# Strassen's seven-product scheme for the two MLP products over pairs of batches, with attention in head pairs and transposed activations

## The chip, the cores and the metric

The kernel runs on one NeuronCore of one Trainium2 chip. The metric is the device time of one execution in microseconds (us); lower is better. TensorE (PE in the profile) multiplies matrices: it loads a stationary tile of weights and streams a moving tile of up to 448 columns here into PSUM. VectorE (DVE), ScalarE (ACT) and GpSimd (POOL) work element by element; DVE and ACT read PSUM. SyncE (SP) only starts transfers in this kernel.

## The reference

Attention over 4 batches, 12 heads, 448 positions and 64 channels per head, then two MLP blocks on the 448x768 activations of each batch. Only the first MLP has a layer norm; the second has a low-rank mixing over the sequence in front of it.

```python
def _attn_ref(q, k, v, g_q, g_k):
    q_n, k_n = (rmsnorm(q, g_q), rmsnorm(k, g_k))
    scores = scale * np.matmul(q_n, k_n.transpose(0, 1, 3, 2))
    attn = softmax(scores)
    return np.matmul(attn, v)
def _moe_ref(x, g_ln, w_ch1, w_ch2):       # w_ch1 768x3072, w_ch2 3072x768
    xn = (x - mu) / np.sqrt(var + 1e-06) * g_ln
    return x + np.maximum(xn @ w_ch1, 0.0) @ w_ch2
def _moe2_ref(x, U, V, w_ch1, w_ch2):      # U 448x32, V 32x448
    u = x + (x.transpose(0, 2, 1) @ U @ V).transpose(0, 2, 1)
    return u + np.maximum(u @ w_ch1, 0.0) @ w_ch2
```

## The kernel before

Precision: each factor of a large product is split into a high part in the format fp32r and the low remainder (`x_hi`, `x_lo`), and a product is the sum of three matmuls, hi x hi, hi x lo and lo x hi. ACT makes a high part by a copy, DVE the low part by a subtraction.

**Attention** (function `attention`) goes head by head, 48 heads, in a loop over pairs of heads whose body `step` is written out for each engine with fixed offsets between the stages (a software pipeline). For each head PE does: 4 transposes of the normalised k (`turn_k`, L333), 4 times two matmuls for the scores (`score`, L296 and L297; q's high and low half are stacked into 128 rows, so two matmuls replace three), 16 transposes of the exponentials (`turn_exp`, L308) and 16 fp32 matmuls with v (`values`, L322; the trace has two records for each). DVE takes the row maxima (`maximum`, L444), the bias (`scale_max`, L452), k's low part (L469), q's low part (L476), half of the copies of the transposed exponentials (`copy_et`, L463), the sums of squares (L486) and the scaled output (L505). ACT does the exponentials (L372), the other copies and the high parts. POOL squares q and k (`square`, L249), takes the power -0.5 (L267) and normalises k (L271). The result stays in SBUF (`x_all`), natural layout: positions on the partitions.

**MLPs** (function `mlps`) run in 8 stages, one batch of one MLP each. A stage needs its input with channels on the partitions: `build_item` (L669) transposes it, ACT and DVE split it into `in_hi` and `in_lo` (L786, L851, L854). The 3072 hidden channels are 24 blocks of 128. For block j, `hidden` (L733) does 6 x 3 matmuls of 128x128 by 128x448 into one PSUM bank, ACT and DVE make `h_hi` and `h_lo` of it (L817, L932), and `output` (L750) does another 6 x 3 that add to six PSUM banks kept for the whole stage. PE computes block j+1's `hidden` ahead of block j's `output`. Weights come from memory for each block (`load_weights`, L98 and L99), and are split by ACT (L781, L782) and DVE (L844, L845) in tiles of 128x768, three blocks ahead. At a stage's end the six banks are copied (`y_out`, L812 and L927), transposed back in the next stage (`back_item`, L680), and added to x (`residual`, L891). The low-rank mixing stands in the stages 1 to 4 (L698, L706). POOL has three instructions in this part. Each engine runs its own list in the order in which it is written; semaphores hold an instruction until what it reads is there.

## Time and profile before

| | |
|---|---|
| device time, median of 3 runs | 1796.21 us (1795.0 to 1798.2) |
| span of the profiled execution | 1794.6 us |
| first matmul of the first MLP stage | at 344.56 us |
| last matmul of the last `output` | at 1784.44 us |
| busy share of PE, DVE, ACT, POOL | 98%, 51%, 39%, 11% |
| matmul records | 10272 |

The span is read as attention up to 344.56 us, the eight stages from there to 1784.44 us (1440 us), and 10 us for the last transposes, sums and stores. Busy shares are an average over these parts. In attention DVE is busy nearly all the time as well; in the MLPs it is so for some 40%.

### The profile page before, as it was taken

To read this page: it belongs to the slowest core of one execution; us is meant where nothing else is said; L and a number is where in the kernel's file an instruction comes from. 1 tells how busy PE (TensorE), PEld (TensorE's weight loads), DVE (VectorE), ACT (ScalarE), POOL (GpSimd) and SP (SyncE) were. 2 spreads that over 40 slices of the span, in tenths; PEclk is the share of its full clock that TensorE was granted. 3 is DMA by queue.
4 is the path that set the end of the run, shared out by engine and by line. 5 is a ranking of instruction groups with operands and counts; after the bars stand their busy time and mean duration, and the time that the engine had idled before them with its cause. 6 is when DMAs were issued, how large, how long until landed. Compare 5 with 4: busy or idle time off the path is not lost.

```text
span 1794.6 us, 29017 instructions
## 1 busy us (share of the span) xinstructions
PE 1766.4 (98%) x10272; PEld 1655.9 (92%) x10272; DVE 913.4 (51%) x1595; ACT 706.3 (39%) x1268; POOL 202.1 (11%) x201
## 2 busy tenths in 40 slices
PE   6999999999999999999999999999999999999998
PEld 5999999899999999999999999999999999999997
DVE  7999999743344444444444444444433433343332
ACT  5777777522333323332333233323222322232221
POOL 6666666000000000000000000000000000000000
PEclk9999999999999999999999999999999999999999
DMA  2222224233333233333333333332433333333320
GB/s 73 69 69 72 68 71 139 87 106 116 113 106 103 93 111 101 106 106 106 105 108 100 102 100 106 106 106 89 138 121 106 97 131 121 106 99 128 121 88 31
DMA packets 205744, 180.41 MB, mean 101 GB/s; under 512 B 12497, under 2 KB 179281, under 8 KB 205649
## 3 DMA queue, kind: packets, MB, share of 16 engines
q1 hardware_dynamic: 203280, 173.51, 30.3%
q10 hardware_dynamic: 2368, 5.51, 0.8%
q8 instruction: 75, 1.23, 0.3%
q14 instruction: 21, 0.16, 0.0%
HBM read 173.48 MB, written 5.51 MB: 100 GB/s over the span
## 4 chain that ended last, share of the span: by engine, by line
PE 80%; DVE 0%; issue 0%; ACT 0%
PE h_ps L733 39%; PE y_ps L750 38%; PE h_ps L680 1%; PE h_ps L669 1%; PE h_ps L698 1%; PE h_ps L706 0%; PE y_ps L658 0%; DVE in_nat L891 0%; ACT in_hi L786 0%; DVE in_lo L854 0%; DVE in_lo L851 0%; DVE y_t L927 0%
## 5 line engine op out<-in xcount | busy, mean ns | idle before, releaser
L844 DVE TENSOR_TENSOR w_lo<-w_raw,w_hi 128x768 fp32r<-128x768 f32 x190 | 182.0, 958 | 674.0 <-ACT w_hi L782 674.0
L750 PE MATMUL y_ps<-h_hi,w_hi 128*128 128x448 f32 x1152 | 424.4, 368 | 0.0
L733 PE MATMUL h_ps<-in_hi,w_hi 128*128 128x448 f32 x1152 | 415.9, 361 | 3.1 <-DVE in_lo L851 1.1
L733 PE MATMUL h_ps<-in_hi,w_lo 128*128 128x448 f32 x1152 | 417.9, 363 | 0.0
L750 PE MATMUL y_ps<-h_hi,w_lo 128*128 128x448 f32 x1152 | 417.8, 363 | 0.0
L750 PE MATMUL y_ps<-h_lo,w_hi 128*128 128x448 f32 x1152 | 417.7, 363 | 0.0
L733 PE MATMUL h_ps<-in_lo,w_hi 128*128 128x448 f32 x1152 | 417.4, 362 | 0.0
L781 ACT ACTIVATE w_hi<-w_raw 128x768 fp32r<-128x768 f32 x189 | 159.7, 845 | 538.1 <-PE y_ps L750 538.1
L817 ACT ACTIVATE h_hi<-h_ps 128x448 fp32r<-128x448 f32 x192 | 104.7, 545 | 380.1 <-PE h_ps L733 338.5
L733 PEld LDWEIGHTS h_ps<-in_hi,w_hi 128*128 128x128 f32 x1152 | 215.6, 187 | 19.1 <-DVE in_lo L851 1.5
L733 PEld LDWEIGHTS h_ps<-in_lo,w_hi 128*128 128x128 f32 x1152 | 216.2, 188 | 15.8
L750 PEld LDWEIGHTS y_ps<-h_lo,w_hi 128*128 128x128 f32 x1152 | 216.7, 188 | 14.0
L750 PEld LDWEIGHTS y_ps<-h_hi,w_hi 128*128 128x128 f32 x1152 | 215.9, 187 | 13.5
L750 PEld LDWEIGHTS y_ps<-h_hi,w_lo 128*128 128x128 f32 x1152 | 216.1, 188 | 13.0
L733 PEld LDWEIGHTS h_ps<-in_hi,w_lo 128*128 128x128 f32 x1152 | 216.1, 188 | 12.4
L845 DVE TENSOR_TENSOR w_lo<-w_raw,w_hi 128x768 fp32r<-128x768 f32 x190 | 180.7, 951 | 0.0
L322 PEld LDWEIGHTS av_ps<-v_nat,e_t 112*112 112x112 f32 x1536 | 172.7, 178 | 5.2
L322 PE MATMUL av_ps<-v_nat,e_t 112*112 112x64 f32 x1536 | 174.2, 257 | 0.0
L782 ACT ACTIVATE w_hi<-w_raw 128x768 fp32r<-128x768 f32 x189 | 156.4, 827 | 0.0
L932 DVE SCALAR_TENSOR_TENSOR h_lo<-h_ps,h_hi 128x448 fp32r<-128x448 f32 x192 | 118.9, 619 | 71.6 <-ACT h_hi L817 70.9
L372 ACT ACTIVATE e_nat<-scores,nbias,rs_all 112x448 f32<-112x448 f32 x192 | 138.0, 721 | 40.3 <-DVE nbias L452 40.2
L444 DVE TENSOR_REDUCE nmax<-scores 112x1 f32<-112x448 f32 x192 | 113.2, 615 | 4.3 <-PE scores L297 1.6
(90 smaller groups left out, 1407.3 us busy)
## 6 DMA issues: line engine op xcount, KB each, us to landing
w_raw<-in_moe_w_ch SPq DMA_DIRECT2D x384, 384.0 KB, 3.8
qk_raw<-in_q SPq DMA_DIRECT2D x48, 112.0 KB, 2.0
qk_raw<-in_k SPq DMA_DIRECT2D x48, 112.0 KB, 2.1
qt_raw<-in_q_t SPq DMA_DIRECT2D x48, 112.0 KB, 2.5
v_nat<-in_v SPq DMA_DIRECT2D x48, 112.0 KB, 2.0
out<-o_nat ACTq DMA_DIRECT2D x12, 336.0 KB, 5.0
out<-in_nat ACTq DMA_DIRECT2D x4, 336.0 KB, 3.1
...
```

Of the source, the lines that this page charges most:

```text
L322: last = nc.tensor.matmul(av_ps[:TP, m * D:(m + 1) * D], e_t[:, m, c, :], v_nat[:, slot, c, :], start=(c == 0), stop=(c == NI - 1))
L372: nc.scalar.activation(e_nat[:, i, :], scores[i][:TP, :S], ACT.Exp, bias=nbias[:, i:i + 1], scale=rs_all[:, ds(g, 1), i:i + 1].rearrange(" ...
L444: nc.vector.reduce_max(nmax[:, i:i + 1], scores[i][:TP, :S], axis=AX, negate=True).then_inc(rawmax_done, 1)
L669: last = nc.tensor.transpose(h_ps[c % 2][:, i * TP:(i + 1) * TP], in_nat[:, i, c * P:(c + 1) * P], ident[:TP, :TP])
L733: last = nc.tensor.matmul(h_ps[j % 2][:, :S], w[:, j % NW, c, :], x[:, c, :], start=(c == 0 and t == 0), stop=(c == DC - 1 and t == 2))
L750: last = nc.tensor.matmul(y_ps[c][:, :S], w[:, j % NW, c * P:(c + 1) * P], x[:, j % 2, :], start=(j == 0 and t == 0), stop=(j == FC - 1 an ...
L781: nc.scalar.activation(w1_hi[:, r], w1_raw[:, r], ACT.Copy)
L782: nc.scalar.activation(w2_hi[:, r], w2_raw[:, r], ACT.Copy).then_inc(w_hi_done, 1)
L817: nc.scalar.activation(h_hi[:, j % 2, :], h_ps[j % 2][:, :S], ACT.Relu).then_inc(hhi_done, 1)
L844: nc.vector.tensor_tensor(w1_lo[:, r], w1_raw[:, r], w1_hi[:, r].bitcast(F32), ALU.subtract)
L845: nc.vector.tensor_tensor(w2_lo[:, r], w2_raw[:, r], w2_hi[:, r].bitcast(F32), ALU.subtract).then_inc(w_lo_done, 1)
L932: nc.vector.scalar_tensor_tensor(h_lo[:, j % 2, :], h_ps[j % 2][:, :S], 0.0, h_hi[:, j % 2, :].bitcast(F32), ALU.max, ALU.subtract).then_i ...
```

## The change

The kernel is rewritten as one function without hardware loops.

**Attention in head pairs.** A step n of 96 takes one quarter of the positions for both heads of a pair. q and k of the two heads lie on the partitions 0 to 63 and 64 to 127. The scores are three terms (hi x hi, hi x lo, lo x hi) of two matmuls each, one on the rows of each head (`score`, L682). One DVE instruction takes the maxima of both heads (L980). The squares, the power and k's normalisation are done once for a pair on POOL, with twice the elements, and POOL now makes q's low part too (L555). DVE adds the layer-norm statistics and the normalisation (L1016, L1034) in this part; PE transposes x and, if needed, the normalised x into the channel layout (`turn_x`, L713), and the results go to scratch tensors in memory (`xres`, `xnrm`). The first stage's inputs are made in the steps 67 to 94. Only six steps overlap with the MLPs.

**MLPs in 4 stages of two batches.** The two batches are the two column blocks of the right matrix, two halves of the contraction its row blocks, and two halves of the output channels the row blocks of the left one: 2x2 blocks, which Strassen's scheme multiplies with 7 block products instead of 8. `G` products (hidden layer) have 3 chunks x 3 terms = 9 matmuls, `M` products (second layer) 2 x 3 = 6. A stage has 12 groups of 7 `G` products and 18 of 7 `M` products; in a cycle of the order 14 `G` products and 21 `M` products alternate, and each stage has six such cycles. Two `G` products of the next pair of groups (`HEAD`) stand ahead of the `M` products. Matmuls of this kind: 6048, against 6912 before.

The scheme needs sums of blocks. Sums of weights (4 for each group, `weight_sum`, L601), of the input (`make_sums`, L568 to L578) and of the hidden layer (`hidden_sums`, L608 to L618) are done on POOL. Then high and low parts of seven weight, seven input and seven hidden blocks are made, ACT the high and DVE the low ones. Products are combined after each from PSUM by DVE: `combine` (five for each `G` group) and `gather` (seven for each `M` group, into `acc` and `u_acc` in SBUF). Six PSUM banks rotate; P2, P3 and P4 are added by PE onto the banks of P1, P5 and P7 once these have been read out. x and the output keep the channel layout, so the transposes of the MLP stages go; the mixing transposes its tiles in the stages 1 and 2 (L748 to L764). Weights are loaded once for two batches.

```diff
@@ the order of the products @@
+P1, P7, P6, P5, P2, P3, P4 = range(7)
+ORDER = {"G": (P1, P7, P6, P5, P2, P3, P4), "M": (P1, P5, P6, P2, P7, P3, P4)}
+ONTO = {P2: P1, P3: P5, P4: P7}
+        for j in range(NJ):
+            for g in (2 * j, 2 * j + 1):
+                prods += [("G", s, g, k) for k in ORDER["G"][HEAD if g == 2 * j and j else 0:]]
+            if j + 1 < NJ:
+                prods += [("G", s, 2 * j + 2, k) for k in ORDER["G"][:HEAD]]
+            prods += [("M", s, j * NM + m, k) for m in range(NM) for k in ORDER["M"]]
@@ PE @@
-                    nc.tensor.matmul(scores[i][:TP, :S], lhs, k_hi[:, slot, :], start=True, stop=False)
-                    nc.tensor.matmul(scores[i][:TP, :S], lhs, k_lo[:, slot, :], start=False,
-                                     stop=True).then_inc(scores_done, 1)
+                    for a, b in ((q_hi, k_hi), (q_hi, k_lo), (q_lo, k_hi)):
+                        for h in range(2):
+                            rows = slice(h * D, (h + 1) * D)
+                            last = nc.tensor.matmul(mm_ps[:TP, 2 * (n % 2) + h, :S], a[rows, t % 2, i * TP:(i + 1) * TP],
+                                                    b[rows, t % 2], start=a is q_hi and b is k_hi, stop=a is q_lo)
+                def product(q):
+                    kind, s, n, k = prods[q]
+                    pe.wait_ge(wlo_done, q + 1)
+                    if before[q] is not None:
+                        read_out(pe, before[q])
...
+                    if kind == "M" and n % NM == 0:
+                        pe.wait_ge(hlo_done, cut(s * NG + 2 * (n // NM) + 1, k))
...
+                        for p, (w, x) in enumerate(((w_hi, x_hi), (w_hi, x_lo), (w_lo, x_hi))):
+                            last = nc.tensor.matmul(bank(q), w[:, q % RING, c * P:(c + 1) * P], x[:, k, c],
+                                                    start=k not in ONTO and c == 0 and p == 0,
+                                                    stop=c == chunks - 1 and p == 2, skip_group_check=k in ONTO)
@@ POOL @@
+                def weight_sum(r, k):
...
+                    if k == P5:
+                        out, in0, in1, op = s1, a21, a22, ALU.add
...
+                    if k == P6:
+                        out, in0, in1, op = s2, s1, a11, ALU.subtract
...
+                    nc.gpsimd.tensor_tensor(out, in0, in1, op).then_inc(sum_done, 1)
+                def hidden_sums(q):
...
+                        nc.gpsimd.tensor_tensor(t_t1, t_c12, t_b11, ALU.subtract).then_inc(th_done, 1)
+                        pool.wait_ge(th_done, 4 * g + 1)
+                        nc.gpsimd.tensor_tensor(t_c12, t_c22, t_t1, ALU.subtract).then_inc(th_done, 1)
@@ DVE @@
-                nc.vector.tensor_tensor(w1_lo[:, r], w1_raw[:, r], w1_hi[:, r].bitcast(F32), ALU.subtract)
-                nc.vector.tensor_tensor(w2_lo[:, r], w2_raw[:, r], w2_hi[:, r].bitcast(F32),
-                                        ALU.subtract).then_inc(w_lo_done, 1)
+                def weight_low(q):
+                    dve.wait_ge(whi_done, q + 1)
+                    w = width(q)
+                    nc.vector.tensor_tensor(w_lo[:, q % RING, :w], weights(q), w_hi[:, q % RING, :w].bitcast(F32),
+                                            ALU.subtract).then_inc(wlo_done, 1)
+                def hidden_low(g, k):
+                    dve.wait_ge(hhi_done, cut(g, k))
...
+                    nc.vector.tensor_tensor(h_lo[:, k, g % 2], src, h_hi[:, k, g % 2].bitcast(F32), ALU.subtract
+                                            ).then_inc(hlo_done, 1)
+                def combine(q):
...
+                        nc.vector.tensor_tensor(t_c22, bank(q), t_c22, ALU.add).then_inc(comb_done, 1)
+                def gather(q):
...
+                    dve.wait_ge(prod_done, q + 1)
...
+                    nc.vector.tensor_tensor(to, bank(q), to, ALU.add).then_inc(ev_done, 1)
```

On PE, in attention, part of one head stood like this before (scores of one head between the values and transposes of its neighbours; `scores`, `et_ps`, `av_ps` are PSUM tiles):

```order
L322 MATMUL av_ps<-v_nat,e_t 112x64 x4
L296 MATMUL scores<-k_hi,q_st 112x448
L297 MATMUL scores<-k_lo,q_st 112x448
L308 MATMUL et_ps<-ident,e_nat 112x112 x4
L322 MATMUL av_ps<-v_nat,e_t 112x64 x4
L333 MATMUL kt_ps<-ident,kn 128x112 x4
L296 MATMUL scores<-k_hi,q_st 112x448
L297 MATMUL scores<-k_lo,q_st 112x448
L322 MATMUL av_ps<-v_nat,e_t 112x64 x4
L308 MATMUL et_ps<-ident,e_nat 112x112 x8
```

On PE, in the middle of attention, one step stands like this now, up to the next step's scores (`mm_ps` holds scores and values, `sc_ps` the transposes):

```order
L682 MATMUL mm_ps<-k_hi,q_hi 112x448 x2
L682 MATMUL mm_ps<-k_lo,q_hi 112x448 x2
L682 MATMUL mm_ps<-k_hi,q_lo 112x448 x2
L702 MATMUL mm_ps<-v,e_t 112x64 x4
L690 MATMUL sc_ps<-ident,e_nat 112x112 x4
L702 MATMUL mm_ps<-v,e_t 112x64 x4
L690 MATMUL sc_ps<-ident,e_nat 112x112 x4
L713 MATMUL sc_ps<-ident,x_nat 128x112 x4
```

All scores of a quarter stand together, each line being two matmuls on the two halves of the rows; values and transposes of the two heads alternate behind them.

On DVE, in the MLP stages, a block of 36 matmuls had this beside it before:

```order
L932 SCALAR_TENSOR_TENSOR h_lo<-h_ps,h_hi 128x448
L844 TENSOR_TENSOR w_lo<-w_raw,w_hi 128x768
L845 TENSOR_TENSOR w_lo<-w_raw,w_hi 128x768
L860 BN_STATS stats<-x_all 112x6 x2
L932 SCALAR_TENSOR_TENSOR h_lo<-h_ps,h_hi 128x448
```

On DVE, at the first `M` products behind two groups of `G` products, this stands now (`h_lo<-ht` is a hidden block's low part, `acc` and `u_acc` are the sums of `gather`):

```order
L1055 TENSOR_TENSOR h_lo<-ht,h_hi 128x448
L1101 TENSOR_TENSOR u_acc<-mm_ps,u_acc 128x448
L1040 TENSOR_TENSOR w_lo<-w_raw0,w_hi 128x256
L1055 TENSOR_TENSOR h_lo<-ht,h_hi 128x448 x2
L1101 TENSOR_TENSOR acc<-mm_ps,acc 128x448
L1040 TENSOR_TENSOR w_lo<-w_raw0,w_hi 128x256
L1101 TENSOR_TENSOR u_acc<-mm_ps,u_acc 128x448
L1055 TENSOR_TENSOR h_lo<-ht,h_hi 128x448
L1101 TENSOR_TENSOR acc<-mm_ps,acc 128x448 x2
```

Between two reads of PSUM there are now up to three subtractions that read two SBUF tiles each, and two of the low parts that the next `M` products need stand behind the read-out of the product ahead of them.

On POOL, where the MLP stages had nothing but one power for a batch, a stretch of one cycle reads now:

```order
L601 TENSOR_TENSOR w_s2<-w_s1,w_raw0 128x384
L601 TENSOR_TENSOR w_s2<-w_raw0,w_s2 128x384
L608 TENSOR_TENSOR ht<-ht 128x448
L610 TENSOR_TENSOR ht<-ht 128x448
L613 TENSOR_TENSOR ht<-ht 128x448
L618 TENSOR_TENSOR ht<-ht 128x448
L601 TENSOR_TENSOR w_raw1<-w_raw1 128x384
L601 TENSOR_TENSOR w_s1<-w_raw0 128x256
```

The sums of weights and of hidden blocks share one queue, each reading SBUF and writing SBUF.

## Rows read from the trace of the kernel before

**Rows 1.** The page's 40 equal slices of the span; digits are busy tenths.
```profile
PE   6999999999999999999999999999999999999998
DVE  7999999743344444444444444444433433343332
POOL 6666666000000000000000000000000000000000
PEclk9999999999999999999999999999999999999999
```

**Rows 2.** The chain that ended last, by line.
```profile
PE h_ps L733 39%; PE y_ps L750 38%; PE h_ps L680 1%; PE h_ps L669 1%; PE h_ps L698 1%; PE h_ps L706 0%; PE y_ps L658 0%; DVE in_nat L891 0%; ACT in_hi L786 0%; DVE in_lo L854 0%; DVE in_lo L851 0%; DVE y_t L927 0%
```

**Rows 3.** Windows: bounds, length, then busy us (instructions) of PE, PEld, DVE, ACT, POOL; clock.
```profile
50.00:300.00 250.00, 250.00 (x2279) 239.71 (x2278) 237.96 (x575) 193.39 (x456) 157.92 (x152) 1.00 0.28 79
1100.00:1300.00 200.00, 200.00 (x1029) 187.22 (x1028) 84.38 (x120) 63.12 (x96) 0.00 (x0) 1.00 0.34 110
```

**Rows 4.** The chain in order of time: start, length, what (the last MLP matmuls).
```profile
1777.60 7.22 PE y_ps L750 x36
```

**Rows 5.** Timeline of PE and DVE: start, length, engine, line (start of work, of the MLPs, end).
```profile
15.53 0.71 PE L296 MATMUL scores<-k_hi,q_st 128*112 128x448 f32 x1 [6.00 <-DVE k_lo L469]
344.56 0.45 PE L733 MATMUL h_ps<-in_hi,w_hi 128*128 128x448 f32 x1
1784.44 0.37 PE L750 MATMUL y_ps<-h_hi,w_lo 128*128 128x448 f32 x1
```

**Rows 6.** Timeline of PE near the end of attention, values and transposes.
```profile
332.91 1.70 PE L322 MATMUL av_ps<-v_nat,e_t 112*112 112x64 f32 x16
334.44 0.93 PE L308 MATMUL et_ps<-ident,e_nat 112*112 112x112 f32 x8
335.97 0.55 PE L308 MATMUL et_ps<-ident,e_nat 112*112 112x112 f32 x4
336.36 2.48 PE L322 MATMUL av_ps<-v_nat,e_t 112*112 112x64 f32 x24
```

**Rows 7.** One line's instructions (q's low part, once a head): durations, first and last start.
```profile
L476 DVE TENSOR_TENSOR q_st<-qt_raw,q_st x48: 618/619/620, 14.1 to 321.6; 64x448 fp32r<-64x448 f32 x48
```

**Rows 8.** Groups by line: count, busy us, mean ns, idle before. DVE and ACT.
```profile
L444 DVE TENSOR_REDUCE nmax<-scores 112x1 f32<-112x448 f32 x192 | 113.2, 615 | 4.3 <-PE scores L297 1.6
L817 ACT ACTIVATE h_hi<-h_ps 128x448 fp32r<-128x448 f32 x192 | 104.7, 545 | 380.1 <-PE h_ps L733 338.5 <-DVE o_nat L891 41.6
```

**Rows 9.** Timeline of DVE and PE in the MLPs: back-to-back pitch, and hand-off from PE.
```profile
725.62 0.49 PE L680 MATMUL h_ps<-ident,y_t 128*112 128x128 f32 x3
726.26 0.56 DVE L891 TENSOR_TENSOR x_all<-h_ps,x_all 112x384 f32 x1 [0.61 <-PE h_ps L680]
754.00 0.96 DVE L844 TENSOR_TENSOR w_lo<-w_raw,w_hi 128x768 fp32r<-128x768 f32 x1 [3.11 <-ACT w_hi L782]
754.87 0.95 DVE L845 TENSOR_TENSOR w_lo<-w_raw,w_hi 128x768 fp32r<-128x768 f32 x1
```

**Rows 10.** Groups by line on POOL.
```profile
L267 POOL TENSOR_TENSOR rs_all<-qk_ms,m_half 112x8 f32 (+1 forms) x47 | 93.0, 1980 | 101.7 <-DVE qk_ms L488 101.7
L271 POOL TENSOR_TENSOR kn<-qk_raw,rs_all 112x256 f32<-112x256 f32 x94 | 55.6, 612 | 8.2 <-POOL rs_all L267 7.0
L249 POOL TENSOR_TENSOR qk_sq<-qk_raw 112x512 f32<-112x512 f32 x47 | 48.9, 1040 | 0.0
```

**Rows 11.** DVE beside POOL: two lines' durations (min/median/max), then one timeline.
```profile
L452 DVE TENSOR_TENSOR nbias<-nmax,rs_all x96: 146/160/724, 20.8 to 333.2; 112x2 f32<-112x2 f32 x96
L436 DVE TENSOR_TENSOR kn<-qk_raw,rs_all x2: 410/832/1253, 6.8 to 8.0; 112x256 f32<-112x256 f32 x2
...
22.80 1.04 POOL L249 TENSOR_TENSOR qk_sq<-qk_raw 112x512 f32<-112x512 f32 x1
...
23.13 0.72 DVE L452 TENSOR_TENSOR nbias<-nmax,rs_all 112x2 f32<-112x2 f32 x1
```

**Rows 12.** Transfers: KB each, median us from issue to landing.
```profile
w_raw<-in_moe_w_ch SPq DMA_DIRECT2D x384, 384.0 KB, 3.8
```

1721 lines of the change are left out of this document (966 added, 755 removed).

## The prediction

> **What bounds the kernel now.** I read the page's slices first: PE is at 9 tenths in every slice but the first and last, at full clock, so the kernel is bound by PE and the clock has nothing to give back [rows 1]. The chain of waits says the same: nearly all of it is PE, and 77% are the two MLP products [rows 2]. Then the windows: in attention PE is busy for all of 250 us and DVE for 238 of them, POOL for 158; in the MLPs PE is busy for all of 200 us, DVE for 84, ACT for 63, POOL not at all [rows 3]. So the MLPs have slack on DVE, ACT and POOL, attention has little on DVE. The MLP matmuls stand at 7.22 / 36 = 0.2006 us each [rows 4], 6912 of them = 1386 us of the 1440 us between 344.56 and 1784.44 [rows 5]; the other 54 us are transposes and the mixing.
>
> **Attention, PE.** From 332.91 on, 16 records of the values take 1.70 us and 24 take 2.48, so 0.0975 each; eight transposes take 0.93, less the last one's tail 0.095 each [rows 6]. One head is 32 x 0.0975 + 20 x 0.095 + 8 x 0.20 = 6.6 us; measured are (321.6 - 14.1) / 47 = 6.54 us [rows 7]. So the unit prices hold, and PE alone sets attention.
>
> A pair now costs 64 x 0.0975 = 6.2, 32 x 0.095 = 3.0 for the exponentials, 11 more transposes (k 4, x 4, normalised x 3 on average) = 1.1, and the scores. These are 12 couples of matmuls, each matmul on one half of the rows. No row shows such a couple. The nearest rows give its ends: 0.20 us if the halves run at once, like one matmul of 128 rows, 0.40 if one runs after the other. I take 0.20: the two use different rows of the array, different banks and no semaphore stands between them, so they ask for what one full matmul asks for. That is 2.4 us a pair, and 12.75 in all. (The Trainium skill, page TensorEngine Tiling (Array Packing), section Key Properties, says that different tiles can load and multiply in parallel, and that a change of tiling mode drains the engine. No run here shows it yet; by it the sum stays at 2.4 and each step pays two drains.)
>
> **Attention, the other engines.** DVE: 768 elements follow each other at 0.87 us [rows 9], and 448 take 0.615 [rows 8] with about 0.53 pitch, so pitch is 0.05 + 1.07 ns per element. A pair needs 4 x (max of 896: 1.01, bias 0.16, copy 0.53) = 6.8, sums of squares 1.4, k's low part 0.6, inverse and output 0.95, statistics and normalisation 2.0: 11.75 us, below PE's 12.75. POOL: 512 elements 1.04, 256 elements 0.61, so 0.18 us + 1.67 ns per element; the power takes 1.98 for 8 columns, so some 3.9 for 16 [rows 10]: 1.9 + 3.9 + 1.0 + 0.9 = 7.7 us, hidden under 12.75. But k's low part stands behind the fourth maximum, the statistics in front of a copy that PE waits for, and the bias waits for POOL's squares now and then (below). I price this at 0.95 us a pair: 13.7. Seven pairs also carry the 21 low parts of the first stage's inputs (21 x 0.53 = 11 us of DVE): 14.3. Sum 17 x 13.7 + 7 x 14.3 = 333 us. Its ends are 24 x 12.75 = 306 (no wait) and 360 (15 a pair). The first score came at 15.53 [rows 5]; the longer power and the saved second q and k pass cancel, 14.5. Some 4 us lie between the last values and the first product. First product: 14.5 + 333 + 4 = 351.5, that is 7 us later than before.
>
> **MLPs, PE.** 6048 x 0.2006 = 1213 us; mixing 12 items x (8 transposes, 8 matmuls of 256 columns, 2 of 448) = 12 x 2.1 = 25 us. Together 1238, against 1440: 202 us less. If nothing else held PE, this is the gain.
>
> **MLPs, DVE and POOL.** DVE by the pitch above: weights' low parts 336 x 0.47 + 504 x 0.33 = 324; hidden low parts 336 x 0.53 = 178; input low parts 63 x 0.53 = 33; `combine` 240 x 0.53 = 127; `gather` 504 x 0.53 = 267; mixing 32; final sums 5. Total 967 us of 1238, 78%; before it was 84 of 200. POOL: weight sums 192 x 0.82 + 288 x 0.61 = 333; hidden sums 192 x 0.93 = 179; input and final sums 63 x 0.93 = 58. Total 570, 46%. ACT: 336 x 0.49 + 504 x 0.37 + 639 x 0.545 by [rows 8] and some = 710, 57%, hidden.
>
> DVE and POOL aren't independent. The bias normally takes 0.16 us, once 0.72: it started at 23.13 and ended at 23.85, and POOL's squares ran from 22.80 to 23.84. At the start DVE's normalisation of k took 0.41 and 1.25, the longer beside the first squares [rows 11]. So a DVE instruction that reads two SBUF tiles waits for a running POOL instruction. DVE's read-outs of PSUM are not known to. (The Trainium skill, page SBUF — State Buffer, section SBUF: two separate sides, calls this an exclusive lock: whichever of a GpSimd operation and a DVE operation with two SBUF inputs starts first holds the shared port for its whole length. The trace agrees, 0.72 against 0.16.) Of DVE's 967 us, 540 are of this kind; with POOL's 570 they fill 1110 of 1238 us, 90%.
>
> The price: in 35 products a cycle, 24 cycles, there are some 840 places where DVE begins a run of such instructions. POOL is at work for 570 / (1238 - 540) = 0.8 of the time outside them, half of 0.76 us is left: 0.3 us each, 250 us. DVE then needs 1217 of 1238. It is nearly a second bound, in a fixed order. What reaches PE: (a) In each cycle the first `M` group's P6 needs a hidden low part that stands behind the read-out of P1, a weight's low part and one wait: 0.15 hand-off [rows 9] + 0.53 + 0.33 + 0.3 + 0.53 + 0.15 = 2.0 after P5 starts, and P5 lasts 1.2. That is 0.8 x 24 = 19 us. (b) Other places where DVE lags, 1.05 a cycle, a judgement: 25 us. (c) Three stage boundaries: 21 input low parts (11 us) meet 25.2 us of `M` products with 18 us of DVE work, +4, and ACT stands at transfers of 896 KB (two of 384 KB land in 3.8 us [rows 12]), +5: 27 us. (d) DVE's mixing in stages 1 and 2: 10 us. Sum 81. Ends: 10 (no collisions matter) and 130 (DVE waits for 60% of POOL's time, below).
>
> **Tail.** Before, 10.2 us from 1784.44 to the end. Now a read-out, three sums and stores of 900 KB: 8 us.
>
> **Sum.** 351.5 + 1238 + 81 + 8 = 1678.5 for the profiled execution. Its span before was 1794.6, the median 1796.2, so 1.6 more: 1680.
>
> **Rivals.**
> 1. Forecast, 1630 to 1720: 0.50.
> 2. PE alone. POOL's sums fall beside DVE's PSUM reads, DVE keeps up. For it: 427 us of DVE's work don't read two SBUF tiles, and DVE has slack. Against: 90% for the shared resource. 340 + 1238 + 15 + 8 = 1601, so 1605: 0.15.
> 3. Score couples run one after the other. PE has 15.15 a pair and waits less, 15.5 x 24 = 372 instead of 333: 1720. For it: no row shows a couple. 0.10.
> 4. DVE becomes the bound: it waits for 60 to 70% of POOL's time. 967 + 342 to 399, plus (a) and (c) 46, plus 359.5 = 1715 to 1772; 1740. For it: the queues are fixed and both engines work without pause. 0.16.
> 5. Slower. DVE and POOL take strict turns in the MLPs, so that DVE waits for all of POOL's time: 967 + 570 = 1537, and 359.5 + 1537 = 1896. It decides from a wait of 1794.6 - 359.5 - 967 = 468 us, 82% of POOL's time. For it: each hidden sum feeds a DVE subtraction. Against: `gather` and `combine` read PSUM. 0.07.
> 6. The change doesn't do what it says (more matmuls than 6048, or two SBUF passes that the prices miss), about no change: 0.02.
>
> **Numbers.** The likeliest is 1680. Cases 2 to 4 reach down to 1600 and up to 1770; beyond stand case 5 and the edges, under 2 in 10. A measurement of this kernel tells 0.2% from no change, 3.6 us. Faster 0.91, same 0.01, slower 0.08.
>
> **What the changed profile would show.** PE's matmuls at 0.20 and 6048 of them. Couples of L682: starts a few ns apart, or 0.2. First product near 350. Among PE's waits, DVE `h_lo` (L1055) and `w_lo` (L1040) ahead of `acc`; L1040, L1055 with a maximum far above the minimum (0.33, 0.53) and the median above it. DVE busy near 95% in the MLPs, POOL near half. Wrong would be: PE waiting for ACT or transfers, POOL's instructions longer than 0.61, 0.82 and 0.93, or attention at over 360 us.

## The result: 11% slower, where 6% faster was forecast

The changed kernel takes 2010.99 us (median of six; 1978.01 to 2078.52), the kernel before 1795.69 in the same series. Executions of one kernel differ by the time that TensorE spends at its lower clock: medians here are of all of them, and the ratio, 1.1083 with a 95% interval of 1.1016 to 1.1151, is that of the fast ones. The forecast was 1680, with a range up to 1770 and a chance of 0.08 for slower. Kernels with the same attention differ in it from one execution to the next as well; that is why the experiments below are read in two parts, split at the first MLP product. The profiled execution is the slowest of the six, 2078.52, and its span is 2076.7. Against the sum for the profiled execution (1678.5) it is 400 us late.

Page of the changed kernel, the 40 slices (tenths busy; PEclk is the granted clock), to be held against [rows 1]:

```profile
PE   7999999989899999778898996899899869999996
DVE  3466884565898889898887888988888888998887
POOL 4233452341454445574454445744444465554552
PEclk9997995565999999999999998899999979999998
```

The chain that ended last, by engine and line, to be held against [rows 2]:

```profile
PE 59%; DVE 32%; issue 5%; POOL 1%; DMA 1%; ACT 1%; SPq 0%; DVEq 0%; POOLq 0%; ACTq 0%
PE mm_ps L735 38%; DVE w_lo L1040 11%; PE mm_ps L702 9%; DVE h_lo L1055 8%; PE sc_ps L690 5%; PE mm_ps L682 4%; DVE in_lo L1049 2%; DVE acc L1101 2%; PE sc_ps L713 1%; DVE nmax L980 1%; DVE ht L1078 1%; PE sc_ps L756 1%; DVE ht L1075 1%; DVE u_acc L1101 1%; DVE ht L1068 1%
```

Before, nearly all of the chain was PE. Now a third is DVE, and its two largest lines are the low parts of weights and of hidden values. Timeline, the places of [rows 5], and the last MLP matmul:

```profile
14.93 0.71 PE L682 MATMUL mm_ps<-k_hi,q_hi 64*112 64x448 f32 x2 [1.59 <-DVE k_lo L972]
...
516.91 0.72 PE L735 MATMUL mm_ps<-in_hi,w_hi 128*128 128x448 f32 x1
...
2069.68 0.36 PE L735 MATMUL mm_ps<-h_hi,w_lo 128*128 128x448 f32 x1
```

The first product comes at 516.8 (its weight load) in place of the forecast 351.5: 165 us of the 400. From there to the end of the span it is 1560 us in place of 1327: 233 us. So both parts are longer, for different reasons. The 165 us belong to the slowest execution: since the MLPs take about 1555 us whatever the attention did (below), the median stands for a first product near 2011 - 2 - 1555 = 454 and the fastest, 1978, for one near 421 (estimates). Windows, as in [rows 3] (length, then busy us and instructions of PE, PEld, DVE, ACT, POOL; clock); the first three are attention, then the MLPs from their first product, and one boundary between stages:

```profile
20.00:120.00 100.00, 100.00 (x505) 85.17 (x504) 43.56 (x85) 37.91 (x93) 30.79 (x18) 1.00 0.12 35
220.00:320.00 100.00, 94.62 (x830) 80.42 (x829) 84.12 (x175) 64.69 (x155) 51.31 (x31) 0.95 0.26 79
320.00:420.00 100.00, 100.00 (x507) 85.96 (x506) 53.60 (x113) 42.99 (x102) 30.54 (x20) 0.50 0.24 72
...
517.00:2068.00 1551.00, 1362.47 (x6305) 1202.63 (x6304) 1336.89 (x2110) 685.02 (x1544) 799.24 (x732) 0.95 0.24 79
...
856.10:904.50 48.40, 31.72 (x114) 26.57 (x114) 41.52 (x58) 16.61 (x37) 32.16 (x28) 0.79 0.32 101
```

**Attention.** In the first and third window PE is busy for every microsecond and does some 505 matmuls in 100 us; in the one between them it has pauses and does 830. In the third window the clock reads 0.50, the lower of the two levels (1.2 GHz). In the first it reads 1.00, but the rate is the same, and so are the durations: the column missed it there, and durations are the safer reading. The same couples of scores in a slow stretch (64 to 71 us) and in a fast one (225 to 233 us); durations are min/median/max in ns:

```profile
L682 PE MATMUL mm_ps<-k_lo,q_hi x4: 572/572/572, 64.9 to 70.9; 64*112 64x448 f32 x4
...
L682 PE MATMUL mm_ps<-k_lo,q_hi x6: 362/363/364, 225.6 to 233.3; 64*112 64x448 f32 x6
```

The maximum of the scores is taken once a step, so its starts count steps. This is the slow stretch, the next fast one, and a fast one of 54 steps in the kernel `m_nopool` below, whose attention is the same:

```profile
L980 DVE TENSOR_REDUCE nmax<-mm_ps x17: 1085/1092/1092, 19.0 to 116.7; 112x2 f32<-112x896 f32 x17
...
L980 DVE TENSOR_REDUCE nmax<-mm_ps x17: 1073/1082/1093, 226.9 to 286.8; 112x2 f32<-112x896 f32 x17
```
```profile
L981 DVE TENSOR_REDUCE nmax<-mm_ps x55: 1071/1091/1092, 28.3 to 224.2; 112x2 f32<-112x896 f32 x55
```

The first of the 16 intervals of the slow stretch is the pipeline's second step, from 19.0 to 21.8. Without it (116.7 - 21.8) / 15 = 6.33 us a step at the lower clock; (286.8 - 226.9) / 16 = 3.74 and (224.2 - 28.3) / 54 = 3.63 at the full one. Four steps are a pair: 25.3 against 14.5 us. The forecast had 13.7.

What PE did before the clock fell can be read as well. Here it waits 2.06 us for k's low part, and a microsecond later the couples take 0.58 in place of 0.37:

```profile
306.25 0.91 PE L702 MATMUL mm_ps<-v,e_t 112*112 112x64 f32 x8
309.23 0.57 PE L690 MATMUL sc_ps<-ident,e_nat 112*112 112x112 f32 x4 [2.06 <-DVE k_lo L972]
...
310.71 0.58 PE L682 MATMUL mm_ps<-k_lo,q_hi 64*112 64x448 f32 x2
```

All three falls of this attention come so: behind a wait of 1.29 us for `e_t` (at 170), this one, and one of 2.87 us for `e_t` (at 460). The low stretches last 114 us (from the first scores on), 31, 126 and 56, together 327; from 20 us on PE is busy within them without a gap. Not every such wait is followed by a fall: `m_nopool` passes one of 1.29 us at 124 at the full clock. In that kernel the same attention has low stretches of 13, 10, 34, 8 and 10 us, 75 in all.

**MLPs.** PE's waits between 540 and 1780 us (total, times, longest):

```profile
PE mm_ps L735 <- DVE h_lo L1055: 59.5, 32, 4.6
PE mm_ps L735 <- DVE acc L1101: 27.5, 6, 6.0
PE sc_ps L756 <- DVE xs_lo L1113: 23.7, 32, 1.7
PE mm_ps L735 <- DVE ht L1073: 17.0, 12, 2.4
```

All four are DVE's. After a long one the clock is down for a while, which is a second price of the same wait:

```profile
852.56 0.37 PE L735 MATMUL mm_ps<-h_hi,w_lo 128*128 128x448 f32 x1
856.91 0.71 PE L735 MATMUL mm_ps<-h_hi,w_hi 128*128 128x448 f32 x1 [3.99 <-DVE h_lo L1055]
857.43 0.57 PE L735 MATMUL mm_ps<-h_lo,w_hi 128*128 128x448 f32 x1
857.80 0.57 PE L735 MATMUL mm_ps<-h_hi,w_lo 128*128 128x448 f32 x1
```

Groups on DVE and POOL between 640 and 1640 us (busy us, mean ns). `acc` reads PSUM, the others two SBUF tiles:

```profile
L1055 DVE TENSOR_TENSOR h_lo<-ht,h_hi 128x448 fp32r<-128x448 f32 x212 | 200.7, 964 | 6.6 <-ACT h_hi L872 6.6
L1101 DVE TENSOR_TENSOR acc<-mm_ps,acc 128x448 f32<-128x448 f32 x234 | 145.4, 621 | 74.8 <-PE mm_ps L735 72.9
L1040 DVE TENSOR_TENSOR w_lo<-w_raw,w_hi 128x256 fp32r<-128x256 f32 x230 | 132.2, 575 | 0.0
...
L608 POOL TENSOR_TENSOR ht<-ht 128x448 f32<-128x448 f32 x30 | 40.6, 1353 | 33.8 <-ACT ht L897 33.8
L618 POOL TENSOR_TENSOR ht<-ht 128x448 f32<-128x448 f32 x30 | 39.7, 1325 | 11.4 <-DVE h_lo L1055 11.4
```

### The profile page after: what moved, and what is told of

The parts are those of the page before. It is cut to its first block, busy times and chain, and to the rows that moved or that the text cites. A ratio compares the mean times of both kernels' runs of the same rounds, so it can differ in the third digit from the quotient of the medians.

```text
span 2076.7 us, 29152 instructions
## 1 busy us (share of the span) xinstructions
PE 1853.1 (89%) x9432; PEld 1620.5 (78%) x9432; DVE 1651.8 (80%) x2745; ACT 934.3 (45%) x2140; POOL 988.7 (48%) x854
## 4 chain that ended last, share of the span: by engine, by line
PE 59%; DVE 32%; issue 5%; POOL 1%; DMA 1%; ACT 1%; SPq 0%; DVEq 0%; POOLq 0%; ACTq 0%
PE mm_ps L735 38%; DVE w_lo L1040 11%; PE mm_ps L702 9%; DVE h_lo L1055 8%; PE sc_ps L690 5%; PE mm_ps L682 4%; DVE in_lo L1049 2%; DVE acc L1101 2%; PE sc_ps L713 1%; DVE nmax L980 1%; DVE ht L1078 1%; PE sc_ps L756 1%; DVE ht L1075 1%; DVE u_acc L1101 1%; DVE ht L1068 1%
## 5 line engine op out<-in xcount | busy, mean ns | idle before, releaser
L735 PE MATMUL mm_ps<-h_hi,w_hi 128*128 128x448 f32 x1008 | 400.0, 397 | 117.8 <-DVE h_lo L1055 79.1
L843 ACT ACTIVATE w_hi<-w_raw 128x256 fp32r<-128x256 f32 (+1 forms) x552 | 239.2, 446 | 379.8 <-POOL w_raw L601 295.4
L735 PE MATMUL mm_ps<-in_hi,w_hi 128*128 128x448 f32 x1008 | 377.3, 374 | 24.0 <-DVE ht L1073 23.5
L735 PE MATMUL mm_ps<-h_lo,w_hi 128*128 128x448 f32 x1008 | 389.2, 386 | 0.0
L735 PE MATMUL mm_ps<-h_hi,w_lo 128*128 128x448 f32 x1008 | 388.8, 386 | 0.0
L735 PE MATMUL mm_ps<-in_lo,w_hi 128*128 128x448 f32 x1008 | 373.2, 370 | 0.0
L735 PE MATMUL mm_ps<-in_hi,w_lo 128*128 128x448 f32 x1008 | 373.0, 370 | 0.0
L1040 DVE TENSOR_TENSOR w_lo<-w_raw,w_hi 128x256 fp32r<-128x256 f32 (+1 forms) x552 | 348.5, 638 | 5.8 <-ACT w_hi L843 5.8
L1055 DVE TENSOR_TENSOR h_lo<-ht,h_hi 128x448 fp32r<-128x448 f32 x336 | 317.5, 963 | 10.1 <-ACT h_hi L872 10.1
L702 PE MATMUL mm_ps<-v,e_t 112*112 112x64 f32 x1536 | 256.0, 330 | 2.6 <-DVE e_t L991 2.6
L601 POOL TENSOR_TENSOR w_raw<-w_raw,w_s 128x256 f32<-128x256 f32 x72 | 59.5, 827 | 328.7 <-DVE w_lo L1040 328.7
```

What stands on the lines that cost most here:

```text
L601: nc.gpsimd.tensor_tensor(out, in0, in1, op).then_inc(sum_done, 1)
L702: last = nc.tensor.matmul(mm_ps[:TP, 4 + t % 2, cols], e_t[h][:, c * TP:(c + 1) * TP], v[:, t % 2, h, c], start=c == 0, stop=c == NI - 1)
L735: last = nc.tensor.matmul(bank(q), w[:, q % RING, c * P:(c + 1) * P], x[:, k, c], start=k not in ONTO and c == 0 and p == 0, stop=c == chu ...
L843: nc.scalar.activation(w_hi[:, q % RING, :width(q)], weights(q), ACT.Copy).then_inc(whi_done, 1)
L1040: nc.vector.tensor_tensor(w_lo[:, q % RING, :w], weights(q), w_hi[:, q % RING, :w].bitcast(F32), ALU.subtract).then_inc(wlo_done, 1)
L1055: nc.vector.tensor_tensor(h_lo[:, k, g % 2], src, h_hi[:, k, g % 2].bitcast(F32), ALU.subtract).then_inc(hlo_done, 1)
```

## The experiments

All are edits of the changed kernel. "First product" and "MLP part" (from it to the end of the span) are from each kernel's profiled execution, in us; "PE" and "DVE" are busy us of windows over the MLP part. "Time" is the median.

| kernel | time | first product | MLP part | PE | DVE |
|---|---|---|---|---|---|
| changed kernel | 2010.99 | 516.8 | 1560 | 1362 | 1337 |
| a_fill2 | 2055.16 | 495.1 | 1555 | | |
| a_fill4 | 2045.94 | 496.1 | 1550 | | |
| a_rows128 | 1998.31 | 443.3 | 1554 | | |
| a_twice | 2038.53 | 479.0 | 1555 | | |
| a_start | 1994.88 | 453.1 | 1556 | | |
| m_nopool | 1856.48 | 408.6 | 1419 | 1313 | 1089 |
| m_memset2 | 1860.83 | 429.6 | 1425 | 1318 | 1093 |
| m_nolow | 1804.03 | 419.3 | 1379 | 1311 | 826 |
| m_neither | 1799.74 | 444.8 | 1354 | 1294 | 697 |
| m_nogather | 1999.43 | 483.5 | 1525 | 1344 | 1153 |
| m_nohid | 1899.96 | 419.2 | 1447 | 1330 | 1200 |
| m_noweight | 1900.09 | 455.9 | 1468 | 1322 | 1216 |
| v_hid_dve | 1973.34 | 422.6 | 1530 | | |
| v_tables | 2029.25 | 427.1 | 1577 | | |
| v_hid_order | 1963.99 | 478.8 | 1520 | 1343 | 1319 |
| v_all_dve | 2005.89 | 437.8 | 1537 | 1346 | 1360 |
| v_start_order | 1951.24 | 422.7 | 1521 | | |
| v_start_late | 1954.94 | 438.1 | 1514 | | |

The six kernels with the changed kernel's MLPs lie within 1550 to 1560. So the split works: 1555 is the MLPs' own figure, whatever the attention did, and differences of under some 10 us between MLP parts, each of one execution, tell nothing.

### Attention: what lets the clock fall and stay down

**a_fill2, a_fill4.** The edit of the first; the second adds one more matmul ahead of each `turn_e`.

```
                     wait(pe, exp_done, 2 * (n - 1))
+                    for h in range(2):
+                        nc.tensor.matmul(mm_ps[:TP, 2 * (n % 2) + h, :S], q_hi[:, t % 2, i * TP:(i + 1) * TP],
+                                         k_hi[:, t % 2], start=True, stop=True)
```

> The changed kernel with two matmuls added to each of the 96 attention steps (128 rows, 448 columns, written to the banks of the scores just before the scores overwrite them); nothing else differs and the output is the same. Theory C (attention falls to the lower clock level because what TensorE does there, 64-row couples, 64-column values and transposes, does not keep the clock up although no gap shows): the 192 additional matmuls cost 192 x 0.2 = 38 us, but the steps of 5.98 us become about 3.8, so the first MLP product starts at 380 to 420 us in place of some 500, and the time is 1900 to 1960. Rival W (attention is late for waits on VectorE and ScalarE, the clock follows): first product 38 to 75 us later than now, time 2040 to 2090.

> As the one with two, with four added matmuls a step (two more ahead of the transposes of the exponentials). Theory C: 77 us of additional matmuls, every step at the full clock, about 4.2 us a step: first product at 410 to 430 us, time 1920 to 1950; closer to full clock than with two, so the clock of the first 400 us reads 0.95 or more. Rival W: first product at 580 or later, time over 2080.

**a_rows128.** `a[rows, t % 2, ...]` and `b[rows, t % 2]` in `score` become `a[:, t % 2, ...]` and `b[:, t % 2]`.

> The six scores of a step read all 128 rows in place of 64 each, as many and as wide as before (the output is then not the reference's: both heads of a pair are summed). Two matmuls of a couple no longer run together, so at the full clock a step needs 6 x 0.2 in place of 3 x 0.2 and some for the scores, 0.5 to 0.6 us more, 50 to 58 us over 96 steps. If the half array is what lets the clock fall (theory C1), the granted clock stays at 1.0 and steps take about 4.1 us: first product at about 400 us, time 1900 to 1960. If the transposes and the narrow values let it fall (C2), the steps stay at half rate and take 5.98 + 1.1 = 7.1 us: first product at 560 to 600 us, time 2080 to 2130.

**a_twice.** `for a, b in ((q_hi, k_hi), ...)` in `score` becomes `for a, b in 2 * ((q_hi, k_hi), ...)`.

> All six 64-row scores of a step are computed twice (the second time from the start again, so the output is the same). A step has 0.6 us more of TensorE work at the full clock, nearly as much as the full-row scores added, but all of it on half arrays. Theory C1 (half-array work is what lets the clock fall): the steps stay at half rate for most of attention, 5.98 + 1.2 = 7.2 us, first product at 560 to 680 us, clock of the first 400 us at 0.5 to 0.8. Theory C3 (too little busy time let it fall): the clock stays at 0.95 or more, steps of 4.1 us, first product at 430 to 450 us as with full rows.

Windows of attention in a_fill2, then a_fill4, a_rows128 and a_twice:

```profile
20.00:120.00 100.00, 95.42 (x629) 78.26 (x627) 55.47 (x99) 45.17 (x111) 34.65 (x20) 0.74 0.16 45
```
```profile
20.00:120.00 100.00, 94.94 (x777) 77.39 (x777) 66.56 (x118) 52.16 (x128) 39.48 (x23) 1.00 0.18 52
220.00:320.00 100.00, 93.24 (x734) 76.30 (x733) 74.33 (x136) 51.17 (x123) 39.29 (x24) 0.95 0.20 63
```
```profile
20.00:120.00 100.00, 91.31 (x773) 86.06 (x772) 73.91 (x130) 57.81 (x142) 44.48 (x25) 0.98 0.19 54
220.00:320.00 100.00, 91.71 (x749) 85.96 (x747) 82.78 (x159) 59.25 (x142) 46.94 (x29) 0.95 0.29 87
```
```profile
20.00:120.00 100.00, 93.28 (x824) 78.82 (x823) 66.51 (x118) 52.20 (x128) 39.81 (x24) 0.95 0.18 52
220.00:320.00 100.00, 91.81 (x797) 78.15 (x797) 76.36 (x143) 53.20 (x127) 41.09 (x26) 0.92 0.21 66
```

With more matmul work in each step three kernels read 0.92 or more in these windows (a_fill2, with the least, 0.74 in its first), and their record counts, 734 to 824, agree; PE is then *less* busy (91 to 95 of 100 us), since it waits for others more often. So the time of the waits isn't what made attention late. But rival W is right that the clock follows waits: in a_fill4 every fall in attention, too, stands behind a wait of 1.02 to 3.1 us for k's low part or `e_t`. What differs is how long it stays down: about 3 us behind the waits of 1.02 (11 behind one of 2.23, 18 behind one of 2.33), against 31 to 126 in the changed kernel. a_twice has nine such falls from 20 us on, of 3 to 14 us; a_fill2 is between, with up to 51. Full rows aren't needed either: the same half-array couples, done twice, hold it (0.95), so C1 in its plain form falls, which had 560 us or more for a_twice's first product; 479 was measured. C3's clock is about right, its 430 to 450 us were too early. What is left is this: the clock falls behind waits, and in attention's own steps it can stay down for long: the longest stretch is 126 us in the changed kernel, 34 in m_nopool, 79 in m_nolow and 76 in m_nogather, all with the same attention. With added matmul work, of whatever kind, it is 51, 18 and 14 us in a_fill2, a_fill4 and a_twice. Why, these runs don't show. The added work costs more than it brings: with two and with four fillers the first product comes at 495 and 496, ahead of the 517 of the changed kernel's slowest execution but behind the 454 of its median, and the times, 2055.16 and 2045.94, are over 2010.99. Theory C had first products of 380 to 420 and 410 to 430 and missed both; a_fill2's time even lies in rival W's range. a_rows128 gets to 443; its steps take (217.1 - 20.1) / 47 = 4.2 us:

```profile
L980 DVE TENSOR_REDUCE nmax<-mm_ps x48: 1073/1091/1092, 20.1 to 217.1; 112x2 f32<-112x896 f32 x48
```

**a_start.** `for _ in range(44): nc.tensor.matmul(sc_ps[1][:, :P], ident[:], ident[:], start=True, stop=True)` ahead of `turn_k(0)`.

> The changed kernel with 44 matmuls of the identity with itself (128 columns, result unused) ahead of the first transposes, in the 12 us in which TensorE has nothing to do. Nothing else differs, the output is the same. Theory I (the idle start decides whether the first steps run at the full clock): every execution has about 187 records per 20 us from the first steps on, first product at 405 to 425 us, time 1965 to 1980 in nearly all executions, a narrower spread than 1978 to 2079. Rival T (the clock falls whenever, by the load of the steps): the same spread as before, 1975 to 2080, with half-rate stretches in the first 120 us as often.

PE's 88 records stand at 1.58 to 14.03, and the first couples of scores take 0.37 us, the full rate. Then PE waits 1.62 us for the first exponentials, and the couples behind that wait take 0.58 us. The next windows, PE alone, are these:

```profile
35.00:55.00 20.00, 20.00 (x103) 0.50 0.16 47
55.00:75.00 20.00, 20.00 (x103) 0.50 0.12 36
75.00:95.00 20.00, 20.00 (x145) 0.75 0.17 46
```

Windows of 20 us at the full clock hold some 187 records. Executions lie between 1979.41 and 2037.82, and the first product comes at 453, not at 405 to 425. Rival T is nearer, with one thing to add: the clock doesn't fall just anywhere but behind a wait, and a warm start is lost at the first one. One and the same code runs either way: kernels with the changed kernel's attention have 92 to 122 records from 15 to 35 us and 103 to 189 from 35 to 55, by execution.

### MLPs: collisions, load, order

**m_nopool** and **m_nolow**; **m_neither** is both.

```
-                    nc.gpsimd.tensor_tensor(out, in0, in1, op).then_inc(sum_done, 1)
+                    few = w if r < 4 else 8
+                    nc.gpsimd.tensor_tensor(out[:, :few], in0[:, :few], in1[:, :few], op).then_inc(sum_done, 1)
...
-                    w = width(q)
+                    w = width(q) if q < 2 * RING else 8
```

The four sums of `hidden_sums` are cut as the first, `h_lo` as the second.

> GpSimd's weight sums and hidden sums in the MLPs write 8 columns in place of 256 to 448 (after the first runs; the output is then not the reference's), so its work hardly overlaps VectorE's two-input subtractions. Theory D (the MLP's excess over TensorE is VectorE's waits beside GpSimd, and GpSimd's own chain): VectorE's subtraction for a 256-column weight block returns to about 410 ns from 640, TensorE's waits on h_lo shrink from 78 us to under 20, the MLP part takes about 1300 in place of about 1550 us, time 1740 to 1800 with the attention as it is. Rival P (TensorE itself sets the MLP's time, by its clock and pitch): VectorE is faster but the time is 1930 to 2000.

> VectorE's subtractions for w_lo and h_lo write 8 columns in place of 256 to 448 after the first ones (so the output is not the reference's), GpSimd's sums stay whole. The MLP part is read from the first product to the end: 1551 us in the changed kernel, 1410 us with GpSimd's sums cut. Theory D1 (the loss is VectorE's and GpSimd's operations hitting each other): both are gone from each other's way, the MLP part takes 1380 to 1420 us as with the sums cut. Theory D2 (the loss is that GpSimd's own three sums in a row come late): GpSimd runs a sum of 448 in 1.15 in place of 1.3 us and little else changes, MLP part 1480 to 1530.

> Both cut: GpSimd's sums and VectorE's w_lo and h_lo write 8 columns (the output is not the reference's). What is left of the MLP part is TensorE with its own pace and the hand-offs. If the pitch of 0.2067 us a matmul in place of 0.2006 is TensorE's own here, 6048 x 0.2067 + 25 = 1275 plus some 15 to 40 of hand-offs and boundaries: 1290 to 1320 us. If the wider pitch comes from the other engines' traffic, it returns to 0.2006 and the MLP part takes 1250 to 1280 us. If the granted clock still falls to 0.95 in the MLP, it is over 1340.

m_nopool brought 1555 - 1419 = 136 us, where 250 were expected: theory D is right in kind, half in size. m_nolow, at 1379, lands on the edge of D1's range, but it takes work off DVE as well as collisions (826 busy us in place of 1337). m_neither comes to 1354. Its PE does the same 6048 products and mixing, in most stretches (here 600 to 700 us) without a pause; over the MLPs it is busy for 1294 us and idle for 51, most of that at the boundaries between stages, which neither cut touches. That puts it over the first two expectations and into the third's "over 1340", though the clock reads 0.98 and not 0.95:

```profile
600.00:700.00 100.00, 100.00 (x495) 92.53 (x495) 46.63 (x158) 51.65 (x117) 10.92 (x56) 1.00 0.22 70
...
445.00:1790.00 1345.00, 1294.15 (x6306) 1172.38 (x6306) 696.87 (x2110) 679.82 (x1544) 229.98 (x732) 0.98 0.28 92
```

**m_memset2.** Sums replaced by two memsets of the output and a sum of 8 columns.

```
+                def set_twice(to):
+                    for _ in range(2):
+                        wait(pool, ms_twice, len(sets))
+                        nc.gpsimd.memset(to, 0.5).then_inc(ms_twice, 1)
+                        sets.append(1)
...
-                    nc.gpsimd.tensor_tensor(out, in0, in1, op).then_inc(sum_done, 1)
+                    set_twice(out[:, 8:])
+                    wait(pool, ms_twice, len(sets))
+                    nc.gpsimd.tensor_tensor(out[:, :8], in0[:, :8], in1[:, :8], op).then_inc(sum_done, 1)
```

> Each GpSimd sum of the MLPs is replaced by two memsets of its output, one behind the other, and a sum of 8 columns (the output is not the reference's). The memset of 128 columns at the start takes 0.20 us, so a hidden sum becomes about 1.2 us as before and GpSimd's chain stays as long, but it reads nothing. The MLP part (first product to the end) takes 1555 us in the changed kernel and 1419 with the sums cut. Theory D1 (the collisions of two-input operations make VectorE late): VectorE's 256-column subtraction goes from 640 to 430 ns if memsets leave it alone, and the MLP part to 1410 to 1440 us. Theory D2 (the length of GpSimd's chain): VectorE gets faster, but the MLP part stays at 1500 us or more. If memsets stop VectorE as the sums do, the run tells nothing between them.

Groups on DVE between 640 and 1640 us, and the window:

```profile
L1081 DVE TENSOR_TENSOR h_lo<-ht,h_hi 128x448 fp32r<-128x448 f32 x224 | 135.0, 621 | 25.8 <-ACT h_hi L898 25.7
L1066 DVE TENSOR_TENSOR w_lo<-w_raw,w_hi 128x256 fp32r<-128x256 f32 x250 | 115.9, 464 | 1.3 <-ACT w_hi L869 1.0
...
640.00:1640.00 1000.00, 917.81 (x4375) 817.49 (x4374) 772.42 (x1469) 477.71 (x1088) 549.56 (x1440) 0.97 0.29 94
```

POOL is busy for 550 of 1000 us, more than the changed kernel's 515, its chain of three hidden sums is as long as before (4.3 us where it was 4.4, near 722 us in both), and DVE doesn't feel it: `h_lo` 621 ns in place of 964. The MLP part is 1425, within 6 us of m_nopool, and theory D1's range is met. The length of GpSimd's chain costs next to nothing; the collisions cost 130 us. (The Trainium skill, page SBUF — State Buffer, section SBUF: two separate sides, has the shared port locked only against a GpSimd operation that reads SBUF. The trace agrees: memsets don't stop DVE.)

**m_nogather.** `to, bank(q), to` in `gather` becomes `to[:, :8], bank(q)[:, :8], to[:, :8]`.

> VectorE's read-out of the second product (gather's addition from PSUM) takes 8 columns in place of 448 (the output is not the reference's). These 504 instructions never waited for GpSimd (620 ns, as ever). Theory Q (VectorE's queue as a whole is the bound of the MLPs, whatever fills it): some 480 x 0.42 = 200 us of its work go, it is no longer the bound, and the MLP part falls from 1555 to 1380 to 1430 us although GpSimd collides as before. Rival L (the collisions lengthen the chain from a first product to the hidden low parts, and only that holds TensorE): the read-outs stand beside that chain, the MLP part stays at 1500 to 1540 us, and TensorE's waits for h_lo stay at 50 us or more.

1337 - 1153 = 184 us of DVE's busy time go and only 30 us of the MLP part. PE's wait for `h_lo` between 540 and 1780 us hardly changes:

```profile
PE mm_ps L735 <- DVE h_lo L1055: 55.2, 31, 4.6
```

Theory Q falls, rival L's figures hold: DVE's total isn't the bound here. A microsecond taken from collided instructions brings three to five times as much (136 us of the MLP part for 248 of DVE's in m_nopool, 108 for 137 in m_nohid, 30 for 184 here).

**m_nohid, m_noweight.** The cut of m_nopool for the hidden sums alone, or for the weight sums alone.

> Of GpSimd's sums only the 192 hidden ones are cut to 8 columns (the output is not the reference's), the 480 weight sums stay whole. With all cut the MLP part is 136 us shorter (1419 against 1555). Theory H (the hidden sums, which lie in the chain from a first product to the hidden low parts, carry the collisions that count): 80 to 110 of the 136 us go, MLP part 1445 to 1475, TensorE's wait for h_lo under 35 us. Rival E (every collision counts by its length; hidden sums are 192 x 1.33 = 255 us of GpSimd's some 700): 35 to 60 us go, MLP part 1495 to 1520.

> The other half: the 480 weight sums are cut to 8 columns (the output is not the reference's), the 192 hidden sums stay whole. Theory H: only 25 to 55 of the 136 us go, MLP part 1500 to 1530, the wait for h_lo stays near 50 us. Rival E: 75 to 100 us go, MLP part 1455 to 1480.

108 and 87 us, together 195, though both at once bring 136. Theory H's range holds for the first and rival E's for the second, so neither theory holds for both. Either kind of collision is enough to make DVE late; that the second adds to a wait that is there already is a reading of the sum, not a thing shown.

**v_hid_dve, v_tables, v_hid_order, v_all_dve.** `hidden_sums` moves from POOL's to DVE's program, ahead of `combine` and `gather`; the tables' first halves become:

```
+        HIGH_AT = ({P3: -2, P2: 1, P5: 1, P6: 2, P7: 2, P4: 5}, {P3: -2, P2: 1, P5: 1, P6: 2, P7: 2, P4: 5})
+        LOW_AT = ({P3: -1, P1: 0, P2: 2, P5: 2, P6: 3, P7: 3, P4: 6}, {P3: -1, P1: 0, P2: 2, P5: 2, P6: 3, P7: 3, P4: 6})
```

v_tables is the tables alone, v_hid_order both, v_all_dve both and `weight_sum` on DVE.

> VectorE computes the hidden sums itself (the same four sums, same output), between the weights' low parts and the read-out that follows; GpSimd keeps the weight sums. VectorE gets 192 x 0.53 = 102 us more work and is rid of the collisions with them. Theory L (not VectorE's total but the collided chain holds TensorE: the read-outs, 200 us of VectorE's work, brought only 31 us): a chain of three sums takes 1.6 in place of 4.0 us, h_lo is on time, MLP part 1440 to 1490 us, time 1870 to 1950 by what the clock does in attention. Rival Q (VectorE's total counts): no gain or a loss, MLP part 1540 to 1600 us.

> The changed kernel with that order alone, the hidden sums still on GpSimd (same output). Theory O: GpSimd's three sums take 4 us, so the earlier place finds them unfinished half of the time and VectorE stands in its queue: MLP part 1520 to 1560, a small gain or none. Rival (order was all of it): 1460 to 1500.

> Hidden sums on VectorE, as in the run v_hid_dve, and besides the high and low parts for P5, P6 and P7 one product earlier in ScalarE's and VectorE's queues, so that those for P6 and P7 stand ahead of the read-out of the first M product (same output). Theory O (after the move the order held the gain: TensorE waited 62 us for h_lo behind that read-out): the waits for h_lo fall under 25 us and the MLP part from 1530 to 1460 to 1490 us. Rival Q (VectorE's load, 86% busy, holds it): waits only change their name, MLP part 1515 to 1540.

> As v_hid_order, and the weight sums on VectorE too (same output). GpSimd has only the inputs' and the final sums left in the MLPs. VectorE's own work is 967 + 102 + 185 = 1254 us by the prediction's prices, over TensorE's floor of 1238, but nothing stops it. Theory C (what collisions cost in the chain is more than the sums cost on VectorE): MLP part 1420 to 1480 us, the shortest with the reference's output. Rival Q (VectorE full): it is the bound at 93% or more busy, MLP part 1500 to 1560.

Only small gains: 25, -22, 35 and 18 us of MLP part. v_hid_dve fell between both theories. In v_all_dve hardly anything collides (`h_lo` 617 ns; POOL is left with 82 us) and yet the MLP part is 1537: DVE is busy for 1360 us of 1528, and PE waits 34 us for `h_lo` and 42 for `xs_lo`. So load does hold PE once it is this high, which m_nogather taken alone would have denied. Rival Q's ranges hold for v_hid_order and v_all_dve. v_tables, the order alone, made it worse, 1577 where 1520 to 1560 was expected; its DVE is busy for 25 us more (1362), and which wait is to blame wasn't followed up.

**v_start_order, v_start_late.** v_hid_order with a_start's matmuls; the second also with a_fill2's from step 56 on.

> The same matmuls at the start, together with v_hid_order (hidden sums on VectorE, low parts ahead of the read-out), output the same. If the two add up: first product at 405 to 425 us, MLP part 1520, time 1925 to 1950. By rival T 1935 to 2010.

> As v_start_order, and two more matmuls a step (448 columns, overwritten by the scores) from step 56 on, where the clock of the last 200 us of attention reads 0.83. They cost 40 x 2 x 0.2 = 16 us. If they hold the clock, the last 40 steps take about 4.2 in place of 5.1 us and the time is 1910 to 1935; if not, 1940 to 1970.

MLP parts of 1521 and 1514 and first products at 423 and 438. v_start_order is the fastest that leaves nothing out, 1951.24 (1921.36 to 1973.75), 60 us less than the changed kernel and still 156 more than the kernel before. The fillers of the second don't hold the clock: behind waits for DVE and ACT it is down again for 31, 20 and 24 us.

## Why the prediction was wrong

**Right.** 6048 MLP matmuls, near 0.20 at full clock; score couples that run together (starts 0.20 apart, rival 3 is out); 14.5 for the first score (14.93). A pair at full clock cost 14.5 us against 13.7, 0.8 x 24 = 19 us in all. **The price of collisions came out within 2 us, by luck in part, and it didn't help:** DVE is busy for 1337 us with the sums and 1089 with them cut, so collisions cost DVE 248 us, where the sum had 250. But the 250 were worked out with 570 us of POOL's time and 0.76 us a sum, and POOL was busy for 799 us with sums of up to 1.35: with the right prices the same working gives more, and m_nopool leaves some collisions in its 1089.

**Step 1 that failed: "the clock has nothing to give back".** It was read from a kernel whose attention keeps PE busy for 250 of 250 us [rows 3], and was carried over to one in which PE waits for k's low part and the exponentials. The prediction saw that wait ("k's low part stands behind the fourth maximum") and priced only its own time, in the 0.95 us a pair; what the clock takes behind it stood at nothing. 165 us of attention's delay: 19 are the pair's price, nearly all of the other 146 come with the lower clock. 50 of the 95 intervals between steps are over 5.5 us, 324 us in all, which is 142 more than 50 x 3.63. And two executions of the same attention bear it out: the changed kernel is at the lower clock for 327 us, m_nopool for 75. 252 us x (1 - 3.63 / 6.33) = 107, and the first products are 516.8 - 408.6 = 108 us apart. That the falls come behind waits is read from the traces, no run took the waits away; why the clock then stays down for 10 or for 126 us in the same code is open. No rival had the clock.

**Step 2: DVE's "own 967".** It used the pitch between queued instructions, 0.53 for 448 columns, and that pitch holds (0.54 in m_nopool). But DVE's work without the sums is the 1089 us of m_nopool, 122 more. The durations of its 2110 instructions add up to 1207 us, so 118 us overlap, at 0.08 each some 1480 instructions; the other 630 stand alone and take their full 0.62, which is 50 us (an estimate; DVE waits some 510 times there). The input low parts, which took 0.92 to 0.98, are 21 more, and the rest wasn't split. DVE's sum is then 1337, over PE's 1238, not 1217 under it.

**Step 3: the stalls, "(a) 19, (b) 25, (c) 27, (d) 10".** PE is idle for 1551 - 1362 = 189 us, not 81. In 48.4 us windows away from boundaries it loses 4.4 each, 142 us over 32 windows; the boundaries and both ends lose 47 more. (a), (b) and (d), 54 us together, stand against the 142; (b), "a judgement", had no row, and for (d), 10 us, PE's waits in the mixing alone are 24 for `xs_lo` and 9 for `mix`. Experiments split the excess: 1354 without collisions and low parts; + 65 for DVE's low parts (1419 against 1354); + 136 for collisions (1555 against 1419).

**Step 4: PE's own 1238.** m_neither's PE is busy for 1294. The pitch is part of it: stretches without waits run at 0.203 (m_neither, 22 starts from 679.67 to 683.93) or at 0.2065 (the changed kernel, 21 starts from 640.17 to 644.30), which is 15 to 36 us on 6048. The rest is put down to matmuls at the lower clock behind waits, where the column reads 0.98; in the changed kernel, at 0.95 and with the wider pitch, PE's busy 1362 us are 68 more.

**Step 5: POOL's prices.** The squares, which read one tile twice, and the broadcast of [rows 10] were poor proxies. With little in their way (m_nolow) sums of two tiles take:

```profile
L613 POOL TENSOR_TENSOR ht<-ht 128x448 f32<-128x448 f32 x34 | 39.6, 1166 | 2.7
...
L601 POOL TENSOR_TENSOR w_raw<-w_raw 128x256 f32<-128x256 f32 x51 | 38.3, 750 | 7.3
```

(1166 - 750) / 192 = 2.2 ns an element, not 1.67, so 1.17 and 0.75 us in place of 0.93 and 0.61. (The Trainium skill, page GPSIMD Engine Reference, section Elementwise — side-by-side cycle accounting, has 4497 ns for 2048 elements, 2.2 ns each; the trace agrees.)

**The rivals.** 4 made DVE the bound of the MLPs by a wait of 60 to 70% of POOL's time; DVE waited for 248 us of 799, 31%, what made it late besides was its own work, and by m_nogather its total alone isn't the bound. 5 ended on the right side with 1537 us for the MLPs (1547 measured without the tail), yet by another way: DVE doesn't wait for all of POOL's 799 us but for 248. That the total, 1896, is the nearest to 2011 is luck. Steps 2 to 5 alone, with attention as forecast, give 351.5 + 1555 = 1907: slower than before without attention's clock.

**Was there ever a gain?** m_neither, with nearly every collision and low part gone from the MLPs, takes 1799.74 against 1795.84 (ratio 0.9982, 0.9928 to 1.0037; its fastest execution 1778.44). Its first product comes 100 us later than before (444.8 against 344.56 in [rows 5]) and its MLPs are 96 us shorter (1354 against 1794.6 - 344.6 = 1450). So the attention apart gives back what is left of the 173 us that 864 fewer matmuls were to save.
